# Reordering the start-up of a three-engine pipeline: one transfer issued earlier, the second tile's preparation dealt out in another order

## The reference

```
scale = min(mag, 0.999) / (mag + 1e-6)          # mag = |a_re + i a_im|
for t in range(S):
    S_re, S_im = a * (S_re + i S_im) + k[t] v[t]^T
    y[t] = q[t] @ S_re
```

## Time and profile before

| | us |
|---|---|
| median of 3 runs | 974.3 |
| the three runs | 974.95, 972.78, 974.3 |
| the profiled execution's own time | 974.95 |
| its span, first to last instruction | 973.2 |
| TensorE busy | 914.6 (94%) |
| VectorE busy | 599.0 (62%) |
| ScalarE busy | 435.9 (45%) |

### The profile page before, as it was taken

One profiled execution on the slowest core, in us unless ns is written; L12 is line 12 of the kernel. 1 busy time (PEld: TensorE's weight loads), 2 busy tenths in 40 slices (PEclk: granted clock), 3 DMA queues, 4 the chain that ended last, 5 costly groups with the idle time before them and its releaser, 6 DMA issues.

```text
span 973.2 us, 14349 instructions
## 1 busy us (share of the span) xinstructions
PE 914.6 (94%) x5352; PEld 806.3 (83%) x5352; DVE 599.0 (62%) x976; ACT 435.9 (45%) x619; POOL 70.5 (7%) x58
## 2 busy tenths in 40 slices
PE   4997749999999999999999999999999999999998
PEld 1555649989989899999899999999788888888887
DVE  4978888999898999899989733356121212121211
ACT  5264353674664664764864654587102020202011
POOL 0000000000000000000000000000222222222221
PEclk9999669999999999999999999999999999999999
DMA  9587291390570570570660540421101010101000
GB/s 335 186 245 220 66 217 59 126 218 24 149 205 14 158 196 13 158 198 14 186 168 13 166 95 9 168 79 40 35 1 65 1 65 0 65 0 65 0 33 33
DMA packets 97878, 99.50 MB, mean 102 GB/s; under 512 B 6928, under 2 KB 88848, under 8 KB 97808
## 3 DMA queue, kind: packets, MB, share of 16 engines
q1 hardware_dynamic: 97808, 98.59, 35.2%
HBM read 63.96 MB, written 29.88 MB: 96 GB/s over the span
## 4 chain that ended last, share of the span: by engine, by line
PE 71%; DVE 16%; ACT 4%; DVEq 3%; DMA 3%; issue 2%; SPq 1%; ACTq 0%
PE ps_p L1347 8%; PE ps L1347 8%; PE ps L1349 8%; PE ps L1348 8%; PE ps_p L1349 7%; PE ps_p L1348 7%; PE ps_ay L1409 4%; PE ps_p L1375 2%; DVE sp L1225 2%; PE ps_ay L1349 2%; PE ps_ay L1347 2%; PE ps_ay L1348 2%; DMA w3s<-in_w3t 2%; PE ps_k L1349 2%; PE ps_k L1347 2%
## 5 line engine op out<-in xcount | busy, mean ns | idle before, releaser
L1347 PE MATMUL ps<-g_h,wo_h 128*128 128x384 f32 x384 | 133.3, 347 | 2.3 <-DVE g_l L1232 2.3
L667 POOL TENSOR_TENSOR abl<-ab,abh 128x512 fp32r<-128x512 f32 x48 | 69.1, 1440 | 895.6 <-DVE abh L1330 895.6
L1349 PE MATMUL ps<-g_h,wo_l 128*128 128x384 f32 x384 | 129.4, 337 | 0.0
L1348 PE MATMUL ps<-g_l,wo_h 128*128 128x384 f32 x384 | 129.3, 337 | 0.0
L1347 PE MATMUL ps_p<-x1h,win_h 128*128 128x384 f32 x336 | 116.8, 348 | 5.8 <-DVE sp L1225 5.8
L1349 PE MATMUL ps_p<-x1h,win_l 128*128 128x384 f32 x336 | 112.7, 335 | 0.0
L1348 PE MATMUL ps_p<-x1l,win_h 128*128 128x384 f32 x336 | 112.5, 335 | 0.0
L1321 DVE TENSOR_TENSOR ab<-ps_ay,bc 128x512 f32<-128x512 f32 x24 | 16.6, 692 | 114.1 <-ACT bc L956 114.1
L776 ACT ACTIVATE sp<-ps_p 128x768 f32<-128x768 f32 (+1 forms) x63 | 46.1, 732 | 86.2 <-PE ps_p L1349 86.2
L789 ACT ACTIVATE g_h<-sp 128x768 fp32r<-128x768 f32 (+1 forms) x71 | 55.4, 780 | 64.4 <-DVE sp L1225 64.0
L1321 DVE TENSOR_TENSOR ab<-ps_p,bc 128x512 f32<-128x512 f32 x24 | 16.6, 692 | 103.2 <-ACT bc L956 103.2
(11 more groups left out here) (167 smaller groups left out, 2028.7 us busy)
## 6 DMA issues: line engine op xcount, KB each, us to landing
qk_scr<-tt SPq DMA_DIRECT2D x16, 576.0 KB, 4.8
stq<-qk_scr SPq DMA_DIRECT2D x48, 192.0 KB, 4.8
qk_scr<-pp SPq DMA_DIRECT2D x16, 576.0 KB, 3.6
stk<-qk_scr SPq DMA_DIRECT2D x48, 192.0 KB, 4.5
an<-in_a_re SPq DMA_DIRECT2D x8, 576.0 KB, 4.0
an<-in_a_im SPq DMA_DIRECT2D x8, 576.0 KB, 5.2
qk<-in_q SPq DMA_DIRECT2D x8, 576.0 KB, 7.5
qk<-in_k SPq DMA_DIRECT2D x8, 576.0 KB, 9.0
```

Source lines behind the costliest of these rows:

```text
L667: tensor_tensor(abl[:, m % AR, :], ab[:, m % 2, :], abh[:, m % AR, :].bitcast(F32), ALU.subtract).then_inc(ab_lo, 1)
L1347: mm(o, wh, xh, start=start, stop=False)
L1348: mm(o, wh, xl, start=False, stop=False)
L1349: return mm(o, wl, xh, start=False, stop=stop)
```

## The change

Nothing is computed in another way; instructions are moved. On SyncE the load of piece 5 stands ahead of tile 1's decays and of tile 0's store of q. On ScalarE the copy of piece 2's low part stands ahead of the first "inverse", the high part of piece 6 ahead of the last low copy, that of piece 7 one group later, and the squares of tile 1's p ahead of `x1_high`. On VectorE "keys end" of tile 0 stands ahead of "m2" of tile 1; all seven "run" steps, the low part of piece 6, "ends" and the first "carry" stand ahead of the first mask (before: five "run" steps); the later pieces are dealt out one to a place; and the two "q" of tile 1 stand ahead of `x1_low` instead of behind "p2".

```diff
@@ SyncE
-            for i in range(3, 5):
+            for i in range(3, 6):
                 load_piece(i)
             wait(prep_p, 2)
             load_a(1)
             store_q(0, first=True)
-            load_piece(5)
             for c in range(NCH):
                 stack_q(0, c)
@@ ScalarE
             w34_rows(4)
+            raw_low_out(2)
             prep_inverse(0)
-            raw_low_out(2)
             w34_rows(5)
...
-            for i in range(4, 6):
+            for i in range(4, 7):
                 raw_high(i)
-                raw_low_out(i - 1)
-            raw_low_out(5)
+                if i <= BY_PE:
+                    raw_low_out(i - 1)
             k_by_tokens(0, 0)
             for i in range(NG):
                 if i + 1 < NG:
                     k_by_tokens(0, i + 1)
                 y_out(0, i, first=True)
-                if i in (0, 2):
-                    raw_high(6 + i // 2)
+                if i == 1:
+                    raw_high(7)
+            prep_psquares(1)
 
             eng.wait_ge(raw_lo, 8)
-            y_loaded(0, 0)
-            x1_high(0, 0, first=True)
-            prep_psquare(1, 0)
-            y_loaded(0, 1)
-            x1_high(0, 1, first=True)
-            prep_psquare(1, 1)
+            for part in range(2):
+                y_loaded(0, part)
+                x1_high(0, part, first=True)
             prep_inverse(1)
@@ VectorE
-                 ["ends"] + steps("carry", 1) + steps("carry", 2, 4) + steps("carry", 8) + steps("carry", 16, 32) + by +
-                 ["p", ("q", 0), ("q", 1), "p2", "inverse", "keys"], first=True)
-            prep(1, False, ["m2"])
-            prep(0, True, ["keys end"])
-            prep(1, False, ["newton", "scale start", "scale"] + steps("a", 0, 1) + steps("run", 1, 2, 3, 4, 5))
+                 ["ends"] + steps("carry", 1, 2, 4, 8, 16, 32) + by + ["p", ("q", 0), ("q", 1), "p2", "inverse", "keys", "keys end"], first=True)
+            prep(1, False, ["m2", "newton", "scale start", "scale"] + steps("a", 0, 1))
+            prep(1, False, steps("run", 1, 2, 3, 4, 5, 6, 7))
+            raw_low(6)
+            prep(1, False, ["ends"] + steps("carry", 1))
             mask_scores(0, 0)
-            between = [steps("run", 6), steps("run", 7), ["ends"] + steps("carry", 1), steps("carry", 2, 4), [], steps("carry", 8),
-                       steps("carry", 16, 32), [], by[:1], by[1:2], by[2:3], by[3:] + ["p"]]
+            between = [steps("carry", 2), steps("carry", 4), steps("carry", 8), steps("carry", 16), steps("carry", 32),
+                       by[:1], by[1:2], by[2:3], by[3:], [], ["p"], []]
             for i in range(NG):
                 if i + 1 < NG:
                     mask_scores(0, i + 1)
                 prep(1, False, between[2 * i])
                 new_state(0, i, ps_z0)
                 prep(1, False, between[2 * i + 1])
-                if i in (1, 3):
-                    raw_low(6 + i // 2)
+                if i == 2:
+                    raw_low(7)
+            prep(1, False, steps("q", 0, 1))
             x1_low(0)
-            prep(1, False, ["p2", ("q", 0), ("q", 1), "inverse", "keys", "keys end"])
+            prep(1, False, ["p2", "inverse", "keys", "keys end"])
```

## The result

| | before | after |
|---|---|---|
| median of 4 runs each | 973.59 us | 982.91 us |
| profiled execution, span | 973.2 us | 981.0 us |
| mean granted clock of TensorE | 0.982 | 0.974 |
| `scores(1, 0)` starts | 139.07 | 148.06 |

The change makes the kernel slower: ratio 1.0097, 95% interval 1.0075 to 1.0118. The direction was forecast, the size was not: +2.7 us and a range up to 981.0 against +9.3 measured, so the prediction was wrong.

A forecast was written before the change was run, and what follows sets the result against it. TensorE, nearly full from `scores(1, 0)` on, was taken to set the time, so start-up delay reaches the end: 2.66 - 2.5 + 2.54 = +2.7 us, from 974.3 to 977.0 us; 8 in 10 within 973.4 to 981.0.

The forecast's parts named there:

- part 2: Groups of attention: VectorE's waits for scores and states fall from 6.6 to 4.1 us, so 2.5 us earlier.
- Part 1: Start-up before the "run" steps: "inverse" starts later and "m2" waits behind "keys end", so "newton" of tile 1 comes 2.66 us later.
- queue rival: Start-up loads: decays land late (+2.0 us) or piece 6 lands 2 to 3 us late; sum +4.7, 979.0 us; chance 0.13.
- a sign that it was wrong: Start-up, 55 to 92 us: any row of ScalarE or VectorE waiting for a transfer would show the prediction wrong.
- I take the middle one: Groups of attention: TensorE's low clock lasts 6 us, the middle of three earlier stretches of 3.5, 6 and 8 us.
- the second rival: Low clock through the groups: 8.2 us of waits, sum +6.8, 981.1 us; with 9 us low, 978.2; chance 0.14.
- Part 3: Tail of the start-up: with "q" moved, VectorE idles between "p2" and "inverse" of tile 1, 2.54 us later.
- Sum at "keys end": End of the start-up: tile 1's "keys end" ends +2.7 us later, at 130.8 instead of 128.1.
- A start-up that hands over later by x makes the end later by x: From `scores(1, 0)` on: TensorE is nearly full, so any delay before it reaches the end in full.
- the prediction's reading of the advice: Groups of attention: by the skill's advice the low-clock term would be nothing and the sum +0.2 us.

The follow-up runs named there:

- e10: The changed kernel once more, unaltered; 983.85 us.
- e3: The kernel before with only VectorE's seven "run" steps, piece 6's low part, "ends" and first "carry" moved ahead of the first mask; 983.15 us, ratio 1.0073.
- e4: The kernel before with only the two "q" ahead of `x1_low` and the squares of tile 1's p ahead of `x1_high`; 976.16 us, ratio 1.0016.
- e9: The kernel before with six "run" steps ahead of the first mask, the seventh behind it, later low parts one mask later; 968.26 us, ratio 0.9939.
- e1: The changed kernel with 38 extra products on TensorE in its idle time before the second scores; 982.49 us, ratio 1.0075 against the kernel before.
- e2: The kernel before with only piece 5's load, piece 2's low copy and tile 0's "keys end" moved as in the change; 977.07 us, ratio 1.0022.
- e8: The changed kernel with VectorE's order in the groups and the high parts of pieces 6 and 7 put back; 978.97 us, ratio 1.0047 against the kernel before.
- e11: The changed kernel with only four "run" steps ahead of the first mask, the others spread between later masks; 976.79 us, ratio 1.0020 against the kernel before.
- e7: The changed kernel with 18 extra products on TensorE ahead of the scores of group 2; 983.22 us.

## Why the prediction was wrong

The prediction had the path and the mechanism: a later first mask, a low clock behind TensorE's idle time, dearer round trips. One term of its sum had the wrong sign, the waits of part 2, because it let the low clock last 6 us where it lasted 25.

- **Part 1, +2.66: right.** "Newton" came at 68.99, forecast 69.0. The queue rival did not occur, but by less than the prediction thought. The decays let ScalarE start the squares at 61.40 (forecast 60.7); they ended at 63.8, and VectorE was free at 63.9: 0.1 us to spare, not 0.8. Piece 6's high part started at 85.55 (84.7) and ended 0.7 us before VectorE reached its low part at 87.69 (87.5), not 1.3. Both rows wait for a transfer, between 55 and 92 us, which the prediction named as a sign that it was wrong. That sign was badly drawn, since its own working has ScalarE wait there; what counts is that VectorE didn't:

```profile
61.40 1.16 ACT L701 ACTIVATE te<-an 128x1152 f32<-128x1152 f32 x1 [2.52 <-DMA an<-in_a_im]
...
85.55 1.48 ACT L684 ACTIVATE wo_h<-raw 128x1536 fp32r<-128x1536 f32 x1 [7.00 <-DMA raw<-in_w_out]
```

- **Part 2, -2.5: wrong, and this is the step that failed.** The first mask came at 91.45 (91.4), the low clock was there, the second mask waited 2.81 (2.7). The failure is in "How long the clock stays low is the unknown ... I take the middle one". It was 25 us, not 6. The term measured 10.0 - 6.6 = +3.4 instead of -2.5, an error of 5.9 in the 6.8 by which the sum was short. I had this case as a rival at a chance of 0.14, with 8.2 us of waits, which was itself 1.8 too few.
- The three lengths I took the middle of weren't alike. The 3.5 and the 6 belong mostly to products of 384 columns, the 8 (some 10 when it is measured from end to end) to the very products that run in these groups, and that was the nearest row. The repeat and the part alone (e10, e3) show that the long stretch is usual for this order, with the one exception in e3. With that row alone I would have been at the 978.2 given under the second rival; no row of before shows 25, and e4 had some 3 with the same products. So the step that failed is to put one length into the sum at all. Why it was 25 stays open.
- **Part 3, +2.54: right in its mechanism, too small.** From the end of "p" to the end of "keys end" it is 15.7 us instead of 12.3, so +3.4: the 2.56 idle before "inverse" as forecast, 0.3 for the last state, which now stands in this stretch, and 0.6 of waiting for the last `x1_high`, itself behind a y that came late out of the slow groups.
- **Sum at "keys end".** 2.7 + 3.4 + 3.4 = +9.5 instead of +2.7. The hand-over moved by 9.0, the span by 7.8 (the shorter low stretch at the hand-over), the medians by 9.3.
- **"A start-up that hands over later by x makes the end later by x": right** in both directions, by e9 and the change, to within 1.7 us: the way from the hand-over to the end is 832.9 to 834.6 us in all nine traces without added products.

The Trainium skill (TensorE: Matmul & The Clock Gate, "What's actually happening") advises not to fit a model to one cold count. The lengths did vary here, from some 3 us to 25. It puts the ramp's penalty at under 1% of a typical kernel's span, and that bound holds here: e1 puts it at 7.2 us, 0.7% of 981. But a bound on the whole span says little about a small change: beside the 9.3 us that this one costs, 7.2 us is no term to leave out, as the prediction's reading of the advice would have it.

## What to carry to other kernels

Where two engines hand small pieces back and forth, the wait that a late first piece puts on TensorE is not paid once: it can take the clock, and then later round trips cost more, long after the wait. Before you queue more work ahead of a hand-over to TensorE, find how long it will stand idle, and if that is near the length behind which your own trace shows the clock falling, spread the work between the hand-overs instead. Short waits alone are no promise of the full clock either (e2, e8, e11). When a length in a trace is to be reused, take it from the stretch that runs the same instructions, and price the longest case too: the same groups had 3 and 10 us of low clock in e4 and in the kernel before.

## What was not expected of the hardware

**The start-up's own switch.** TensorE waits for w3 near 21 to 24 us, and the 32 products that follow took either 10.59 or some 12.28 us. Products of the kernel before and of e8:

```profile
23.84 10.59 PE L1375 MATMUL ps_p<-wo2s,w3s 128*128 128x384 f32 x32 [2.19 <-DMA w3s<-in_w3t]
```

```profile
24.11 12.28 PE L1372 MATMUL ps_p<-wo2s,w3s 128*128 128x384 f32 x32 [3.07 <-DMA w3s<-in_w3t]
```

The granted clock from 24.2 to 28 was 1.00 behind waits of 1.90 to 2.38 us (before, after, e4, e7, e9, e10) and 0.55 to 0.63 behind waits of 2.66 to 3.39 us (e1, e2, e3, e8, e11). By "newton" these five are 1.6 to 2.8 us late: 1.7 is the products' own, the rest is that they start up to 1.1 us later. So behind the longer waits 1.7 us are lost on top of the wait itself. It was seen in five of the eleven traces; which of the other runs have it isn't known, and the medians above hold it in unknown shares.

**The clock falls behind short waits too.** The wait was 4.17 us in the kernel before, but 1.83 us in e8, 1.85 in e2 and 1.58 in e11, and in these three it fell when TensorE was at work again. What decides how long it then stays low, with small products that keep the engine busy, is open: near 3 us in e4, 10 in the kernel before, in e2 and in e8, 25 in the changed one.

**Added instructions cost elsewhere.** From hand-over to end the kernels without added products took 832.9 to 834.6 us (nine traces), those with 18 and 38 took 835.4 and 840.4. The cause was not tried.
